# Moving VectorE's weight sums, GpSimd's token halves and one ScalarE copy in a seven-product matmul

## What is computed

```python
def reference(**kwargs):
    attn_out = _attn_ref(**attn_kwargs)          # q pooled in pairs, softmax, times v
    x = attn_out.transpose(0, 2, 1, 3).reshape(B * S, H * D)     # 1152 tokens x 512
    x = _moe_ref(x=x, **moe_kwargs)
    return _moe2_ref(x=x, **moe2_kwargs)

def _moe_ref(x, w_gate, w_val, w_out):           # w_gate, w_val 512 x 1536, w_out 1536 x 512
    gate = 1.0 / (1.0 + np.exp(-(x @ w_gate)))
    val = x @ w_val
    return gate * val @ w_out
```

## Time and profile before

| | us |
|---|---|
| three runs | 1245.37, 1245.39, 1246.44 |
| median | 1245.39 |
| the profiled execution | 1245.24 |
| its span, first to last instruction | 1243.5 |
| TensorE busy (7618 matmuls) | 1232.9 |
| VectorE, ScalarE, GpSimd busy | 804.0, 594.0, 628.2 |

### The profile page before, as it was taken

How to read it: one execution, slowest core, us unless ns; L and a number is a source line. 1 busy time by engine, 2 the same in 40 slices (tenths; PEclk the granted TensorE clock), 3 DMA queues, 4 the chain that set the end, 5 groups by cost and what they waited for, 6 DMA issues and landing times.

```text
span 1243.5 us, 19917 instructions
## 1 busy us (share of the span) xinstructions
PE 1232.9 (99%) x7618; PEld 1129.9 (91%) x7618; DVE 804.0 (65%) x1682; ACT 594.0 (48%) x1239; POOL 628.2 (51%) x512
## 2 busy tenths in 40 slices
PE   8999999999999999999999999999999999999999
PEld 7888888899999899999998998998998998998998
DVE  7999999988873144776576476476466466466444
ACT  7999999954433344344353243243243233233221
POOL 6577777727763375654254254254254254254221
PEclk9999999999999999999999999999999999999999
DMA  6767667401112331221222222222222222222112
GB/s 172 120 116 124 120 120 120 90 24 34 52 35 68 111 94 52 68 85 52 69 69 67 69 74 64 68 70 66 67 70 68 67 69 69 62 76 68 52 34 93
DMA packets 98911, 95.37 MB, mean 77 GB/s; under 512 B 14528, under 2 KB 73152, under 8 KB 98816
## 3 DMA queue, kind: packets, MB, share of 16 engines
q1 hardware_dynamic: 98496, 93.77, 30.2%
q10 hardware_dynamic: 320, 0.33, 0.1%
HBM read 88.59 MB, written 2.40 MB: 73 GB/s over the span
## 4 chain that ended last, share of the span: by engine, by line
PE 88%; ACT 6%; DVE 4%; issue 2%; DMA 0%; ACTq 0%; POOL 0%; DVEq 0%; POOLq 0%
PE bank L1247 13%; PE bank L1249 13%; PE bank L1248 13%; PE bank L1500 11%; PE bank L1501 11%; PE bank L1502 11%; PE bank L1132 5%; PE bank L1105 4%; PE bank L1145 3%; PE bank L1146 3%; ACT probs L1609 2%; ACT pT_hi L1528 2%; PE bank L1215 1%; PE bank L1216 1%; PE bank L1214 1%
## 5 line engine op out<-in xcount | busy, mean ns | idle before, releaser
L2192 DVE TENSOR_TENSOR c<-bank,c 128x256 f32<-128x256 f32 (+1 forms) x448 | 197.1, 456 | 280.6 <-PE bank L1249 274.1
L1035 POOL TENSOR_TENSOR w_lo<-w_raw,w_hi 128x512 fp32r<-128x512 f32 x128 | 163.7, 1299 | 287.7 <-ACT w_hi L1528 287.7
L1501 PE MATMUL bank<-w_lo,h_hi 128*128 128x512 f32 x578 | 225.2, 390 | 0.0
L1500 PE MATMUL bank<-w_hi,h_hi 128*128 128x512 f32 x578 | 225.1, 390 | 0.0
L1502 PE MATMUL bank<-w_hi,h_lo 128*128 128x512 f32 x578 | 224.4, 388 | 0.0
L1805 ACT ACTIVATE h_hi<-c 128x256 fp32r<-128x256 f32 (+1 forms) x256 | 112.5, 445 | 160.5 <-DVE c L2192 160.2
L1502 PEld LDWEIGHTS bank<-w_hi,h_lo 128*128 128x128 f32 x578 | 108.5, 188 | 22.9
L1528 ACT ACTIVATE c<-bank 128x256 f32<-128x256 f32 (+1 forms) x64 | 26.2, 410 | 214.2 <-PE bank L1249 214.2
L1500 PEld LDWEIGHTS bank<-w_hi,h_hi 128*128 128x128 f32 x578 | 108.6, 188 | 20.8
L1961 DVE TENSOR_REDUCE part_min<-bank 128x1 f32<-128x256 f32 (+2 forms) x216 | 114.7, 558 | 19.3 <-PE bank L1146 12.5
L1501 PEld LDWEIGHTS bank<-w_lo,h_hi 128*128 128x128 f32 x578 | 108.6, 188 | 20.1
(11 more groups left out here) (206 smaller groups left out, 3142.8 us busy)
## 6 DMA issues: line engine op xcount, KB each, us to landing
w_raw<-in_moe_w SPq DMA_DIRECT2D x64, 512.0 KB, 3.6
w_raw<-in_moe_w SPq DMA_DIRECT2D x64, 256.0 KB, 3.1
q_raw<-in_q SPq DMA_DIRECT2D x30, 288.0 KB, 4.8
k_raw<-in_k SPq DMA_DIRECT2D x30, 288.0 KB, 8.5
wo_raw<-in_moe_w_out SPq DMA_DIRECT2D x16, 384.0 KB, 3.3
v_raw<-in_v SPq DMA_DIRECT2D x16, 288.0 KB, 4.8
gv_raw<-in_moe_w_gate SPq DMA_DIRECT2D x12, 256.0 KB, 2.9
gv_raw<-in_moe_w_val SPq DMA_DIRECT2D x12, 256.0 KB, 3.6
```

The lines of the kernel that those rows point to most:

```text
L1035: ins = nc.gpsimd.tensor_tensor(w2_lo[:, u % 2, c], w2_raw[:, c], f32(w2_hi[:, u % 2, c]), ALU.subtract)
L1500: nc.tensor.matmul(dst, hh, wh, start=(first and c == 0), stop=False)
L1501: nc.tensor.matmul(dst, hh, wl, start=False, stop=False)
L2192: nc.vector.tensor_tensor(dst[:, 0:w], bank[:, (u + b) % 3, 0:w], other[:, 0:w], ALU.add).then_inc(done, 1)
```

## The change

Four edits, all in this stretch.

- `sw_sums_24` of the next chunk, on VectorE, moves from the end of the even unit to its begin, ahead of values(u-1); for chunk 4, in unit 0, it stays at the end.
- `sw_hi_rest` (ScalarE) and `sw_lo_rest` (GpSimd) of the next chunk move from the odd unit to the even one; for chunk 4 they stay in unit 1. On GpSimd they now stand ahead of sh_lo_part(u-1).
- `st_lo_part` subtracts its two blocks in two instructions.
- In unit 0 ScalarE's s1_copy stands ahead of sw_hi_raw.

```diff
+        def splits_sums(f, n):
+            return f + 1 in SEVEN and n == (f == SEVEN[0])
...
             def st_lo_part(n, j, nth):
-                at = (slice(None), slice(2 * j, 2 * j + 2))
                 pool.wait_ge(st_hi_done, nth + 1)
-                nc.gpsimd.tensor_tensor(st_lo(n)[at], xs[n][at], f32(st_hi(n)[at]),
-                                        ALU.subtract).then_inc(st_lo_done, 1)
+
+                for c in (2 * j, 2 * j + 1):
+                    ins = nc.gpsimd.tensor_tensor(st_lo(n)[:, c], xs[n][:, c], f32(st_hi(n)[:, c]), ALU.subtract)
+                ins.then_inc(st_lo_done, 1)
...
                 if n == 0 and f + 1 in SEVEN:
                     sw_lo_raw(f + 1)
+                if splits_sums(f, n):
+                    sw_lo_rest(f + 1)
                 if n == 0 and u >= 1:
                     sh_lo_part(u - 1)
-                if n == 1 and f + 1 in SEVEN:
-                    sw_lo_rest(f + 1)
...
+                if u == 0:
+                    s1_copy(u)
                 if n == 0 and f + 1 in SEVEN:
                     sw_hi_raw(f + 1)
-                s1_copy(u)
+                if u >= 1:
+                    s1_copy(u)
                 if u >= 1:
                     gates(u - 1)
-                if n == 1 and f + 1 in SEVEN:
+                if splits_sums(f, n):
                     sw_hi_rest(f + 1)
...
                 f, n = seven(u)
+                if n == 0 and splits_sums(f, n):
+                    sw_sums_24(f + 1)
                 if u >= 1:
                     values(u - 1)
...
-                if n == 0 and f + 1 in SEVEN:
+                if u == 0:
                     sw_sums_24(f + 1)
```

## The result

| | median us | lowest to highest | runs |
|---|---|---|---|
| before | 1245.53 | 1245.20 to 1246.48 | 6 |
| after | 1250.64 | 1249.20 to 1251.41 | 6 |

The ratio is 1.0038 with a 95% interval of 1.0025 to 1.0051: 3.1 to 6.4 us slower. The forecast was 1249.2, slower. The median lies 1.4 above it and 0.3 above the upper end of the range; the forecast's +3.97 us lies inside the interval of the difference.

The account below looks back on a forecast made before the run. The prediction took TensorE, busy 1232.9 of 1243.5 us, as the bound. It added 2.83 us up to P3 of unit 2 and 1.14 behind it, +3.97, to the profiled 1245.24: 1249.2 us, range 1246.8 to 1250.3.

Parts of the forecast that it names:

- The ceiling of 3.0 us: All TensorE losses in the stretch of the seven products, 0.24% of the time, taken as the most any gain could be.
- The rule of turns: VectorE's and GpSimd's SBUF operations alternate, each blocking the other whole; summed to +4.0 us by these turns.
- Units 4, 6, 8: VectorE's two moved sums each wait for a GpSimd subtraction, so P3 loses 1.05 us in each unit.
- Unit 2: VectorE's moved sums wait for GpSimd's pair of sums and its 1.29 us subtraction, so P3 comes 1.97 us later.
- The doubtful 0.86 of unit 1: GpSimd's pieces hold up VectorE's sums of chunk 4, the second ending 0.86 us later; 0 kept as low end.
- What the move gives back: P3 of units 3, 5, 7, 9 on time; behind P3 of unit 2 the old run lost 2.08 us, the new 3.22.
- The sum: Whole stretch: 2.83 + 1.14 = +3.97 us, added to the profiled 1245.24 us, gives 1249.2 us.
- Nothing else moves the time: GpSimd's earlier conversions, SyncE's earlier loads and ScalarE's reordered conversions in the stretch were taken to add no time.
- VectorE's second sum is let through: Rival: in units 2, 4, 6, 8 the second sum goes ahead of GpSimd's subtraction; -0.85 us, 1244.4 us; 10%.
- nothing is blocked: Rival: GpSimd's subtraction falls elsewhere, only unit 2 waits for GpSimd's pair; -1.33 us, 1243.9 us; 6%.
- The third: Rival: partly blocked, unit 2 as forecast and three chunks once only, or the reverse; +0.5 to +2.4 us, 1245.7 to 1247.7; 5%.
- the fourth: Rival: GpSimd becomes the bound, its pair behind VectorE's sum in units 4, 6, 8; each 0.5 to 1 us more; 4%.

Follow-up runs that it names:

- the PSUM run: Changed kernel with VectorE's two weight sums reading an idle PSUM bank in place of one SBUF input: 1243.73 us, ratio to before 0.9974 to 0.9994.
- VectorE's sums only: Against the changed kernel: only VectorE's sums stay moved to the chunk's begin; splits back in the odd unit, no halves, no copy: 1250.32 us, one run.

## Why the prediction was right, point by point

- **The ceiling of 3.0 us and the account of losses.** The account of start times explains the difference of the stretches to 0.04 us (4.03 against 3.99), where the waits of the profile alone say 5.3 - 0.9 = 4.4. No kernel gained as much as the ceiling allows: the best two still lose 1.23 and 1.39 of the 3.0 us.
- **The rule of turns.** Right in each of the five pairs of sums: 1.55, 0.87 and three of about 1.24 for the first, 0.85 and four of 1.40 for the second. I had written "near 1.2" and "near 1.3 to 1.5". The run with one SBUF input shows the blocking as the cause. This agrees with the Trainium skill's rule that such an operation and one of GpSimd shut each other out for the whole instruction (SBUF — State Buffer, section "SBUF: two separate sides"): a sum that takes 0.41 us alone took up to 1.69 beside GpSimd. Whether the engines strictly take turns, or the instruction issued earlier goes first, the rows cannot tell, since in every place GpSimd's was also the one issued earlier. For this sum both come to the same.
- **Units 4, 6, 8:** forecast 1.05 each (its own two figures, 7.23 and 6.16, make it 1.07), measured 1.03, 1.01, 1.00; alone, without halves and copy, 1.00, 1.00, 1.01.
- **Unit 2:** forecast +1.97 in a kernel whose unit 1 is as before; the run with the moved sums alone has 2.00 - 0.07 = 1.93.
- **The doubtful 0.86 of unit 1.** I took the order in which the second sum is held up. It is what happened: losses up to P3 of unit 1 are 1.80 us against 0.86, 0.94 more. With the 0.86 of the forecast at its low end of 0, the sum would have been 0.9 too small. It was a choice between close cases: GpSimd's piece is ahead of the first sum by 0.04 us after the change and by 0.02 or 0.03 in the three experiments with halves or copy. The order was the same in all four, but the prediction could not know that, so this part is in some measure luck.
- **What the move gives back,** 2.08 us behind unit 2, was right: units 3, 5, 7, 9 lost nothing, as unit 11 had shown.
- **The sum** +3.97 against +3.99 in the account and +4.03 in the stretch. Two small misses cancel in it: up to P3 of unit 2 the change lost 2.94 us (forecast 2.83), behind it 1.05 (forecast 1.14).
- **What the sum left out.** "Nothing else moves the time" did not hold. The measured median is 1.4 us above the forecast and 0.3 above the upper end of the range. By the means of the six runs the kernels are 4.7 us apart (1245.76 and 1250.50), not 4.0. The three runs of the changed kernel with the full clock have a mean of 1249.94, 4.2 above before, which is nearly the account; the three with a reduced clock have 1251.06. So the clock, which the sum had at nothing, accounts for most of the 0.7, as far as so few runs can say. The rest of the gap to the forecast is its start from one profiled execution, 1245.24 us, which lies 0.3 under the median and 0.5 under the mean of before.
- **The rivals** that VectorE's second sum is let through, or that nothing is blocked, are refuted for this kernel by the rows at 309.04, 315.98 and 328.16. The second one's price was tested by the PSUM run: 1.23 us lost against 3.00, 1.8 less, where the rival's figure was 1.33 less with unit 0 as before. The third, that some sums are blocked only once, did not come either: all five pairs are blocked twice. Nor did the fourth: GpSimd's own pair for unit 4 ran at 323.76 and 324.46, long before VectorE's sum at 326.89.

## What to carry to other kernels

Before a VectorE operation with two SBUF inputs is moved into idle time of VectorE, look at what GpSimd does there: a hole of 1.1 us did not hold 0.84 us of work, since each of two sums waited for one GpSimd instruction. Two such operations in a row cost two GpSimd instructions; put them where GpSimd itself waits for someone. And making an instruction ready earlier can cost time, since it may then take its turn ahead of one that somebody waits for. When a change makes TensorE wait longer at once, look also at its granted clock, run by run: one profile can miss it.

## What the runs showed of the hardware

- Back to back operations of VectorE do not keep GpSimd out: GpSimd's instruction, issued while the first ran, went ahead of a second that was issued 0.03 us behind the first one's end, in all five places after the change; it was also the one issued earlier, so the rows do not tell turns from order of issue. The operation that waits ends 0.28 us behind GpSimd's (128x256, 0.41 to 0.43 us alone).
- With one operand in PSUM the same 128x256 subtraction takes 0.41 to 0.43 us beside GpSimd: 5 pairs, none held up, and GpSimd's instruction ran beside each of the ten.
- Where in GpSimd's instruction the operation arrives sets its price: issued 0.91 us behind its start (306.31 against 305.40, before) the first sum took 0.85 us, issued 0.04 behind (307.45 against 307.41, after) 1.55. Edits that shift one engine by some 0.5 us (the halves, the copy) changed the order of turns and by the account cost more than they brought.
- After a wait of 1.73 us and 1.3 us of work TensorE's granted clock fell to 0.50 for 3.4 us and cost 1.5 us (VectorE's sums only). In the changed kernel, whose profile shows a wait of 1.80 us and the full clock, it was reduced in three of six runs: the same program has it in some executions and not in others.
